# Moving the split of the MLP's four late weight pieces from VectorE to ScalarE and GpSimd

## What is computed

```python
def _moe2_ref(x, w_in, w_out):          # x 1536x512, w_in 512x2048, w_out 2048x512
    h = x @ w_in
    g = np.where(h > 0.0, h, np.exp(np.minimum(h, 0.0)) - 1.0)
    return g @ w_out
```

## Time and profile before

| | us |
|---|---|
| three executions | 626.35, 629.75, 629.32 |
| their median | 629.32 |
| profiled execution: span from first to last instruction | 626.3 |
| PE busy | 546.3 (87%) |
| DVE busy | 332.7 (53%) |
| ACT busy | 196.8 (31%) |
| POOL busy | 96.3 (15%) |

### The profile page before, as it was taken

One profiled execution on the slowest core, in us unless ns is written; L12 is line 12 of the kernel. 1 busy time (PEld: TensorE's weight loads), 2 busy tenths in 40 slices (PEclk: granted clock), 3 DMA queues, 4 the chain that ended last, 5 costly groups with the idle time before them and its releaser, 6 DMA issues.

```text
span 626.3 us, 9325 instructions
## 1 busy us (share of the span) xinstructions
PE 546.3 (87%) x3292; PEld 486.5 (78%) x3293; DVE 332.7 (53%) x765; ACT 196.8 (31%) x486; POOL 96.3 (15%) x91
## 2 busy tenths in 40 slices
PE   2899997899259899999827979999999999999996
PEld 2688887888159798989716859988898898979985
DVE  6846653455538658688933784343343334343332
ACT  2556654555012122222302232232223222232222
POOL 1001100000034225343730350010000200000000
PEclk9999998999669999999985999999999999999999
DMA  7258896551116748989724110030000200010001
GB/s 159 71 161 248 233 317 224 149 181 68 38 35 199 271 168 287 316 315 329 262 63 155 68 32 19 2 100 2 1 0 13 88 0 0 0 52 2 0 1 50
DMA packets 56968, 73.26 MB, mean 117 GB/s; under 512 B 20640, under 2 KB 26784, under 8 KB 56928
## 3 DMA queue, kind: packets, MB, share of 16 engines
q1 hardware_dynamic: 52448, 64.37, 32.0%
q0 software_dynamic: 1840, 6.03, 3.2%
q10 hardware_dynamic: 2640, 2.38, 1.1%
HBM read 58.09 MB, written 14.68 MB: 116 GB/s over the span
## 4 chain that ended last, share of the span: by engine, by line
PE 47%; DVE 10%; issue 6%; DMA 6%; ACT 2%; POOL 0%; DVEq 0%; POOLq 0%; ACTq 0%
PE ps_g L1134 19%; PE ps_out L1134 19%; DMA xg<-tokens,source_i 5%; PE ps_y L1134 4%; PE ps_h L1323 4%; DVE w_hi L426 3%; DVE w_lo L428 2%; DVE g_raw L1108 1%; ACT g_hi L770 1%; DVE h_lo L1063 1%; DVE g_lo L1111 1%; DVE g_raw L1105 1%; ACT g_raw L766 1%; DMA row_sb<-slots,slot_i 1%; PE ps_x L1293 1%
## 5 line engine op out<-in xcount | busy, mean ns | idle before, releaser
L1134 PE MATMUL ps_g<-x_hi,w_hi 128*128 128x384 f32 x256 | 87.4, 341 | 1.5 <-DVE x_lo L1097 1.5
L1134 PE MATMUL ps_g<-x_lo,w_hi 128*128 128x384 f32 x256 | 87.2, 341 | 0.0
L1134 PE MATMUL ps_g<-x_hi,w_lo 128*128 128x384 f32 x256 | 87.1, 340 | 0.0
L1105 DVE TENSOR_SCALAR g_raw<-g_raw 128x384 f32<-128x384 f32 x64 | 23.0, 360 | 119.7 <-ACT g_raw L766 119.7
L1134 PE MATMUL ps_out<-w_hi,g_hi 128*128 128x512 f32 x192 | 76.7, 399 | 7.9 <-DVE g_lo L1111 7.9
L1162 PE MATMUL ps_qk<-k_pair,q_pad 128*128 128x288 f32 (+1 forms) x192 | 61.4, 407 | 22.2 <-DMA v_sink<-in_v 21.2
L1134 PE MATMUL ps_out<-w_lo,g_hi 128*128 128x512 f32 x192 | 75.8, 395 | 0.0
L1134 PE MATMUL ps_out<-w_hi,g_lo 128*128 128x512 f32 x192 | 75.5, 393 | 0.0
L421 POOL TENSOR_TENSOR w_lo<-raw,w_hi 128x1024 fp32r<-128x1024 f32 x24 | 59.7, 2491 | 88.0 <-ACT w_hi L415 88.0
L766 ACT ACTIVATE g_raw<-ps_g 128x384 f32<-128x384 f32 x64 | 31.4, 491 | 122.0 <-PE ps_g L1134 122.0
L1323 PEld LDWEIGHTS ps_h<-xg_t,up_w 128*128 128x128 f32 x576 | 67.2, 196 | 2.0 <-issue 1.3
(11 more groups left out here) (136 smaller groups left out, 793.6 us busy)
## 6 DMA issues: line engine op xcount, KB each, us to landing
raw<-in_moe_w SPq DMA_DIRECT2D x16, 1024.0 KB, 5.5
up_w<-in_moe_w SPq DMA_DIRECT2D x16, 1024.0 KB, 9.7
raw<-in_moe_w_in SPq DMA_DIRECT2D x4, 1024.0 KB, 5.3
raw<-in_moe_w_out SPq DMA_DIRECT2D x4, 1024.0 KB, 5.3
slots<-zeros SPq DMA_DIRECT2D x2, 1792.0 KB, 7.6
q_pad<-in_q SPq DMA_DIRECT2D x16, 192.0 KB, 3.4
k_pair<-in_k SPq DMA_DIRECT2D x16, 192.0 KB, 3.5
v_pad<-in_v SPq DMA_DIRECT2D x16, 192.0 KB, 3.6
```

The source lines that it names most:

```text
L1105: dve.tensor_scalar(g_raw[f % 2][:], g_raw[f % 2][:], 1.0, 1.0, ALU.min, ALU.subtract).then_inc(g_min_done, 1)
L1134: last = pe.matmul(to, w, x, start=start and m == 0, stop=stop and m == 2)
```

## The change

The four late pieces are no longer touched by DVE. ACT makes `w_hi` of both halves, one half per tile at f = 2 to 9, between the tile's exponential and the copy to `g_hi`. POOL makes `w_lo` of both halves, each when its `w_hi` is there. Nothing else in the order of any queue is changed: POOL's gathers for the second block still stand behind its splits.

```diff
+        LATE = NPX + 2 * NP
+        def late_half(f):
+            return LATE + (f - 2) // 2, f % 2
+        def split_late_act(act, n, half, end):
+            if half == 0:
+                piece_in(act, n, end)
+            cols = slice(half * HALF, (half + 1) * HALF)
+            act.activation(flat(w_hi[place(n)])[:, cols], flat(raw[n % RAW])[:, cols],
+                           ACT.Copy).then_inc(hi_a if half == 0 else hi_b, 1)
+        def split_late_pool(pool, n, end):
+            piece_in(pool, n, end)
+            for half in range(2):
+                cols = slice(half * HALF, (half + 1) * HALF)
+                pool.wait_ge(hi_a if half == 0 else hi_b, n + 1)
+                pool.tensor_tensor(flat(w_lo[place(n)])[:, cols], flat(raw[n % RAW])[:, cols],
+                                   flat(w_hi[place(n)])[:, cols], ALU.subtract).then_inc(lo_a if half == 0 else lo_b, 1)
...
                 if t == TB - 1:
-                    for n in range(NPX + 2 * NP, NPALL):
-                        split_pool(pool, n, end)
+                    for n in range(LATE, NPALL):
+                        split_late_pool(pool, n, end)
...
                     act.activation(g_raw[f % 2][:], ps_g[f % 2][:, 0:TW], ACT.Exp).then_inc(g_exp_done, 1)
+                    if first and 2 <= f < 2 + 4 * NP:
+                        split_late_act(act, *late_half(f), end)
                     act.wait_ge(g_ready, s + 1)
                     if not first or f >= 2:
                         act.wait_ge(g_down_done, s - 1)
                     act.activation(g_hi[f % 2][:], g_raw[f % 2][:], ACT.Copy).then_inc(g_hi_done, 1)
-                    if first and 2 <= f < 2 + 2 * NP:
-                        split_act(act, NPX + 2 * NP + f - 2, end)
...
                     dve.tensor_tensor(g_lo[f % 2][:], g_raw[f % 2][:], g_hi[f % 2][:],
                                       ALU.subtract).then_inc(g_lo_done, 1)
-                    if first and 2 <= f < 2 + 2 * NP:
-                        split_dve(dve, NPX + 2 * NP + f - 2, end)
```

## The result

The changed kernel took 635.6 us in the median (632.76 to 637.73, 15 runs), the kernel before 629.72 us (626.35 to 634.16, 15 runs). The ratio is 1.0083, with a 95% interval from 1.0063 to 1.0104: slower by 5.2 us (4.0 to 6.5). The forecast was 4.2 us and 633.5, with the range 629.5 to 636.5; it stood on a median before of 629.32 from three runs.

What follows compares the result with a forecast made beforehand. PE was taken as the bound, with anything it loses in the first MLP block reaching the end: -3.88 (waits) + 6.0 (gather) + 0.1 (restart) + 2.0 (clock) = +4.2 us on 629.3, so 633.5; range 629.5 to 636.5.

Steps and rivals of the forecast that it cites:

- ACT for nothing: Tiles 2 to 9: ACT's eight halves of 1.04 us cost the chain nothing, hidden behind minimum and maximum; margin 0.08 us.
- POOL holds `g_lo`: POOL's 2.40 us subtraction starts before DVE's `g_lo` and holds it, about 2.3 us instead of 0.56.
- its list of signs: Expected trace signs: long `g_lo` in tiles 2 to 9, PE waits, DVE idle 7.5 us, PE idle 6 us, half-clock matmuls.
- Waits in every second tile: PE waits 0.5 us every second tile, two tiles taking 8.96 instead of 8.36; down(8) 3.88 us early.
- The gather: Behind POOL's last split, it holds DVE's combine 7.5 us; PE stands 6.0 us, down(9) starts 2.25 us late.
- The clock: PE's 6.0 us stand before down(9) brings half clock for 3.0 to 5.9 us, losing 1.4 to 2.7; taken 2.0.
- Sum: Whole kernel: -3.88 + 6.0 + 0.1 + 2.0 = +4.2 us, 633.5 us on the median; chance 0.52.
- without the fall of the clock: Rival: clock stays high through PE's 6 us stand or falls too late to matter; +2.2 us, 631.5; chance 0.17.
- without the hold of `g_lo`: Rival: POOL doesn't hold `g_lo`, so no waits up to tile 8; +2.5 us, 631.8; chance 0.13.
- The late gather: Rival: gather lands 0.6 and issues 0.8 later, full 5.9 us at half clock; +6.3 us, 635.6; chance 0.11.

Runs made afterwards that it cites:

- experiment 6: Kernel before, with POOL setting the first half of the four late pieces' `w_lo` to zero instead of subtracting, reading nothing from SBUF; ratio 0.9928, 4.5 us faster.
- experiment 1: Changed kernel with POOL's three gathers for the second block issued ahead of the late splits; ratio 0.9941, 3.7 us faster than the kernel before.
- experiment 2: Kernel before with only POOL's gathers moved ahead of the late splits; ratio 1.0003 against the kernel before.
- experiment 3: Changed kernel with 22 unused matmuls on PE between up(10) and down(9); ratio 1.0044, 2.8 us slower than the kernel before.
- experiment 8: Changed kernel, gathers first, each POOL subtraction taking the half ACT made one tile earlier and starting behind the minimum; ratio 0.9908, 5.8 us faster than before.

## Why the prediction was right

Against the forecast, all from down(1) in one trace:

- **ACT for nothing.** Right. ACT's half ran from 348.49 to 349.54 and `g_hi` started 1.51 us behind the exponential (348.11 to 349.62), as before. The margin was as thin as stated.
- **POOL holds `g_lo`.** Right: 2.26 to 2.38 us in tiles 2 to 8; forecast 2.35. In tile 9 it took 0.56 us, since DVE came to it behind the gather, with POOL's splits over. The prediction's sum has it so (2.10 us from the minimum to the end of `g_lo`); its list of signs, which names tiles 2 to 9, doesn't. This is the rule of the Trainium skill (SBUF — State Buffer, Who interferes with whom) that no row of before could show for `g_lo`; the traces agree with it for the pair of a subtraction with two SBUF inputs and a reading POOL, and experiment 6 for the other half of the rule, that a POOL instruction which only writes does not take part.
- **Waits in every second tile.** Right: four waits of 0.34 to 0.46 us, and two tiles take 9.1, 9.0 and 9.0 us; forecast 8.96. Down(8) was 3.65 us early; forecast 3.88. That difference doesn't reach the end, for down(9) waits for the gather.
- **The gather.** Right, and shown by experiments 1 and 2. POOL's last subtraction ended 35.30 us behind down(1); forecast 35.27. DVE took 3.86 us from the gather's beginning to the combine, not 3.63. Down(9) was 2.52 us late; forecast 2.25. Of the 0.27 between them 0.23 is this later landing, for which the prediction had bounds from 0 to 1.4 and took 0.
- **The clock.** Right, and shown by experiment 3. From down(9) to down(10) there were 6.43 instead of 4.18 us, so 2.25; forecast 2.0. The mechanism was forecast, the size was the middle between two rows far apart (1.4 and 2.7 us); that it came within 0.25 us is partly luck.
- **Sum.** 4.77 us in the trace, 5.2 (4.0 to 6.5) on the runs; forecast 4.2. The rivals without the fall of the clock (2.2) and without the hold of `g_lo` (2.5) lie outside the interval, and each one's mechanism was seen not to occur. The late gather (6.3 us, 635.6) lies inside the interval of the runs, and its 635.6 is even the measured median. There the trace decides: 0.23 us of its 1.4 came true, and the clock cost 2.25 us, not 2.7. The median agrees with it by chance; the three runs before had a median 0.4 us under that of the fifteen.

One thing the prediction didn't ask, though it cost it nothing. It read that DVE's 3.38 us were POOL's doing, and then priced only what leaves DVE. By experiment 6 POOL's reading was the whole of the 6.2 us in the kernel before. The change took the load off the engine that was held, and left the one that held it, with twice the work.

## What to carry to other kernels

When a step is moved to another engine's queue, look at what stands behind it there. Here three small DMA issues behind the splits were worth 8.4 us of the stretch, since a third engine had its wait for them in the middle of its own order, and PE's clock fell on top. When GpSimd and VectorE both read SBUF, ask which of the two starts first in each tile and what that does to the chain; with the gathers first, the move alone won 3.6 us of the stretch (experiment 1), and with the long instruction placed where its hold fits the slack 5.9 (experiment 8). And a start that is tied to the end of the held instruction can feed back on itself: sum it over tiles, not for one.

## What the runs showed of the hardware that I had not expected

A short hold grows: with POOL's 2.4 us subtraction started behind `g_lo`, DVE's minimum went from 0.36 to 0.71, 1.05, 1.44, 1.77 and 2.14 us in successive tiles. And 22 matmuls whose result nobody uses made the stretch 2.3 us shorter than without them: the granted clock stayed at 1.00 through what was a 6 us wait.
